# Ten query chunks laid at one stride per half, and one load of v's rows per head and half

## The reference, cut to what matters

```python
q_d, k_d, v_d = (mean over groups of 4 positions)          # 144 pooled positions
out_up = np.repeat(sm_attn(q_d, k_d, v_d), 4, axis=2)
mask = np.abs(pos[:, None] - pos[None, :]) < 4
scores = np.where(mask, scale * q @ k.T, -1e9)
out_local = softmax(scores) @ v
x = (out_up + out_local) as 1152 x 512
x = elu(x @ w_in) @ w_out                                  # 512 -> 2048 -> 512
out = sum over 4 experts e of p[:, e] * (relu(x @ w1[e]) @ w2[e])   # 512 -> 1024 -> 512
```

## Time and profile before

| | us |
|---|---|
| median of 3 runs | 653.45 (652.56 to 657.57) |
| the profiled execution | 653.07 |
| its span | 651.3 |
| PE busy | 635.3 |
| DVE / ACT / POOL busy | 348.7 / 283.2 / 321.7 |

### The profile page before, as it was taken

How to read it: one execution, slowest core, us unless ns; L and a number is a source line. 1 busy time by engine, 2 the same in 40 slices (tenths; PEclk the granted TensorE clock), 3 DMA queues, 4 the chain that set the end, 5 groups by cost and what they waited for, 6 DMA issues and landing times.

```text
span 651.3 us, 13151 instructions
## 1 busy us (share of the span) xinstructions
PE 635.3 (98%) x4775; PEld 587.2 (90%) x4775; DVE 348.7 (54%) x764; ACT 283.2 (43%) x786; POOL 321.7 (49%) x278
## 2 busy tenths in 40 slices
PE   8759999999999999999999999999999999999998
PEld 5649999999999999998998898899899899889986
DVE  5657464646557876764544454454365355365342
ACT  4667474848395686564133142152052152142210
POOL 3456444444398799899336238047056064160200
PEclk9789999999999999999999999999999999999999
DMA  8585171614122121302103003012012022010012
GB/s 168 117 218 145 49 183 30 175 33 135 66 65 105 55 99 64 130 1 82 48 2 130 1 7 123 0 53 76 0 64 64 0 64 64 0 65 2 0 49 97
DMA packets 52003, 46.10 MB, mean 71 GB/s; under 512 B 32128, under 2 KB 34432, under 8 KB 51968
## 3 DMA queue, kind: packets, MB, share of 16 engines
q1 hardware_dynamic: 50784, 45.35, 23.4%
q10 hardware_dynamic: 1184, 0.30, 0.2%
HBM read 43.27 MB, written 2.36 MB: 70 GB/s over the span
## 4 chain that ended last, share of the span: by engine, by line
PE 91%; SPq 5%; DMA 1%; ACT 1%; issue 1%; DVE 0%; DVEq 0%
PE psum L538 16%; PE psum L540 16%; PE psum L539 16%; PE psum L609 11%; PE psum L613 11%; PE psum L611 11%; PE psum L679 2%; PE psum L678 2%; PE psum L677 2%; SPq L330 2%; SPq L333 2%; DMA wa_raw<-in_moe_w_in 1%; SPq L312 1%; SPq L316 1%; PE psum L530 1%
## 5 line engine op out<-in xcount | busy, mean ns | idle before, releaser
L1635 POOL TENSOR_TENSOR wb_lo<-wb_raw,wb_hi 128x512 fp32r<-128x512 f32 x64 | 81.8, 1295 | 180.6 <-ACT wb_hi L918 180.6
L1445 DVE SCALAR_TENSOR_TENSOR o_acc<-psum,gate_now,o_acc 128x512 f32<-128x512 f32 x72 | 54.1, 751 | 126.0 <-PE psum L540 125.7
L540 PE MATMUL psum<-wb_hi,h_lo 128*128 128x512 f32 x288 | 112.3, 390 | 0.0
L539 PE MATMUL psum<-wb_lo,h_hi 128*128 128x512 f32 x288 | 112.2, 390 | 0.0
L538 PE MATMUL psum<-wb_hi,h_hi 128*128 128x512 f32 x288 | 112.0, 389 | 0.0
L1028 ACT ACTIVATE h_hi<-psum 128x320 fp32r<-128x320 f32 (+1 forms) x128 | 52.4, 411 | 87.4 <-DVE psum L1417 40.3
L1635 POOL TENSOR_TENSOR wa_lo<-wa_raw,wa_hi 128x512 fp32r<-128x512 f32 x60 | 77.5, 1318 | 16.9 <-ACT wa_hi L959 16.9
L1034 ACT COPY sums<-psum 128x256 f32<-128x256 f32 (+1 forms) x32 | 12.8, 400 | 155.2 <-PE psum L613 155.1
L613 PE MATMUL psum<-x_hi,wa_lo 128*128 128x256 f32 (+2 forms) x228 | 67.4, 296 | 0.0
L611 PE MATMUL psum<-x_lo,wa_hi 128*128 128x256 f32 (+2 forms) x228 | 67.3, 295 | 0.0
L609 PE MATMUL psum<-x_hi,wa_hi 128*128 128x256 f32 (+2 forms) x228 | 67.3, 295 | 0.0
(11 more groups left out here) (192 smaller groups left out, 1670.2 us busy)
## 6 DMA issues: line engine op xcount, KB each, us to landing
wa_raw<-in_moe_w_in SPq DMA_DIRECT2D x8, 1024.0 KB, 5.5
wb_raw<-in_moe_w_out SPq DMA_DIRECT2D x8, 1024.0 KB, 5.0
wa_raw<-in_moe_w SPq DMA_DIRECT2D x8, 1024.0 KB, 5.0
wb_raw<-in_moe_w SPq DMA_DIRECT2D x8, 1024.0 KB, 5.0
out<-o_acc SPq DMA_DIRECT2D x9, 256.0 KB, 2.0
q_in<-in_q SPq DMA_DIRECT2D x10, 144.0 KB, 5.3
v_in<-in_v SPq DMA_DIRECT2D x5, 288.0 KB
v_win<-in_v SPq DMA_DIRECT2D x20, 64.0 KB, 2.8
```

What stands on the lines that cost most here:

```text
L539: nc.tensor.matmul(bank_cols, w_hi(n), x_lo_(n), start=False, stop=False)
L540: last = nc.tensor.matmul(bank_cols, w_lo(n), x_hi_(n), start=False, stop=(n == chunks - 1))
L1445: nc.vector.scalar_tensor_tensor(o_acc[:, m, :], psum[:, DOWN2_BANKS[(MT * half + m) % 2], :], gate_now[:, m:m + 1], o_acc[:, m, :], ALU.m ...
L1635: nc.gpsimd.tensor_tensor(lo[:, c, :], raw[:, c, :], hi[:, c, :].bitcast(F32), ALU.subtract).then_inc(lo_ready, 1)
```

## The change

The five windows of each half now all begin at the same distance of 58. `WIN_SECOND`, 280, is where the second half's first window begins, and the last one ends at 576 exactly. The first chunk of the first half takes 61 tokens, since nothing lies before position 0, the last of the second half 61 as well, and their neighbours at the middle 53 each (tokens 235 to 287, and 288 to 340). The other six keep 58. The places that a chunk's output takes in PSUM follow from its tokens (`at`). Since all five windows of a half fit one access pattern, `load_v` issues four window DMAs of 64 x 5 rows in place of eight, and the wait in `mix` goes by 64 in place of 128.

```diff
-TOK_AT = [HALF * (s % 2) + QSTEP * (s // 2) for s in range(NQT)]
-TOK_N = [min(QSTEP, HALF - QSTEP * (s // 2)) for s in range(NQT)]
-Q_AT = [min(t, SEQ - QT) for t in TOK_AT]
-WIN_AT = [min(max(t - FACTOR + 1, 0), SEQ - WIN) for t in TOK_AT]
+WIN_SECOND = SEQ - WIN - QSTEP * (CHUNKS - 1)
+WIN_AT = [WIN_SECOND * (s % 2) + QSTEP * (s // 2) for s in range(NQT)]
+Q_AT = [0 if s == 0 else min(WIN_AT[s] + FACTOR - 1, SEQ - QT) for s in range(NQT)]
+TOK_AT = [HALF * s if s < 2 else WIN_AT[s] + FACTOR - 1 for s in range(NQT)]
+TOK_N = [(TOK_AT + [HALF, SEQ])[s + 2] - TOK_AT[s] for s in range(NQT)]
...
-                for e, (i0, odd) in enumerate(((1, 0), (0, CHUNKS - 1))):
-                    part = slice(WIN * e, WIN * (e + 1))
+                for e in range(2):
                     for h in range(2):
-                        at = rows.offset + h * SEQ * HD
-
-                        sp.dma_start(win[part, i0:i0 + CHUNKS - 1, h, :],
-                                     bass.AP(rows.tensor, at + WIN_AT[2 * i0 + e] * HD,
-                                             [[HD, WIN], [QSTEP * HD, CHUNKS - 1], [1, HD]])).then_inc(win_loaded[held(u)], 16)
-                        sp.dma_start(win[part, odd, h, :],
-                                     bass.AP(rows.tensor, at + WIN_AT[2 * odd + e] * HD, [[HD, WIN], [1, HD]])
-                                     ).then_inc(win_loaded[held(u)], 16)
+                        sp.dma_start(win[WIN * e:WIN * (e + 1), :, h, :],
+                                     bass.AP(rows.tensor, rows.offset + (h * SEQ + WIN_SECOND * e) * HD,
+                                             [[HD, WIN], [QSTEP * HD, CHUNKS], [1, HD]])).then_inc(win_loaded[held(u)], 16)
...
-                pe.wait_ge(win_loaded[held(u)], 128 * loads(u))
+                pe.wait_ge(win_loaded[held(u)], 64 * loads(u))
...
-                        rows = slice(WIN * e, WIN * (e + 1))
+                        rows, at = slice(WIN * e, WIN * (e + 1)), TOK_AT[c] - HALF * e
...
-                        last = nc.tensor.matmul(psum[HD * h:HD * (h + 1), banks[e], QSTEP * i:QSTEP * i + TOK_N[c]],
+                        last = nc.tensor.matmul(psum[HD * h:HD * (h + 1), banks[e], at:at + TOK_N[c]],
```

## The result

| | before | changed |
|---|---|---|
| median, us | 653.45 (652.56 to 657.57) | 643.73 (643.49 to 643.83) |
| profiled execution, us | 653.07 | 643.81 |
| its span | 651.3 | 642.0 |
| PE busy | 635.3 | 632.8 |

Both medians are now of five executions. The ratio is 0.9846, with a 95% interval of 0.9817 to 0.9876: 9.7 us by the medians, 9.3 us by the two profiled executions. The forecast was 642.3, in a range of 640.0 to 646.8.

A forecast was written before the change was run, and what follows sets the result against it. SP's issuing was taken to bound the first 45 us, PE the rest. Gains of 4.7 + 5.2 + 1.3 = 11.2 us took the profiled 653.07 to 641.9, a median of 642.3, range 640.0 to 646.8.

The forecast's parts named there:

- What binds: Claim that SP's issuing, not a computing engine, bounds the first 45 us, and PE bounds the kernel after that.
- The price of an issue: SP's queue: each new window DMA of 64 x 5 rows takes 0.67 us to issue, bounds 0.57 and 1.34.
- Term A: Up to ACT's `x_hi`: pair 3's q in time, PE's 3.0 us wait and lower clock gone, ACT 4.7 us earlier.
- Term B: At ACT's first weight cast: `wa_raw` lands before ACT wants it, so its whole 5.2 us wait goes; at worst 3.
- Term C: Behind the first weight cast: PE's clock stays up for the products and `mix(3)`; 1.3 us, between 0 and 1.6.
- The sum: Whole kernel: 4.7 + 5.2 + 1.3 = 11.2 us gained, for a median of 642.3 us.
- the signs that the prediction named: Profile after: issues 0.67 us apart, `wa_raw` issued at 26 to 28, `first_wa(0)` near 35, no q wait, full clock.
- Rival 1: First stage: transfers bind, not issues; `wa_raw` lands at 37 to 40, gain 6 to 9 us; chance 0.13.
- Rival 2: SP's queue: a 64 x 5 issue costs what two did, 1.34 us, so time stays 653; chance 0.07.
- Rival 3: `load_v` ahead of `wa_raw`: five-window transfers stall SP, slower, 664 us at 2.0 us an issue; chance 0.03.

The follow-up runs named there:

- experiment 1: Changed kernel's new chunks, but each half's windows loaded in two DMAs again, eight a pair: 653.60 us against 653.72 for the kernel before.
- experiment 2: Changed kernel with window loads merged only for pairs 0 and 1 and the mixed pairs, those of pairs 2 and 3 in eight DMAs: 650.44 us, before 653.72.
- experiment 3: Changed kernel with window loads merged only for pairs 2 and 3, those of pairs 0, 1 and the mixed pairs in eight DMAs: 647.78 us, before 653.72.
- experiment 4: The changed kernel itself once more, with no edit: 643.75 us against 653.72 for the kernel before.
- experiment 6: Changed kernel with the first weights issued ahead of pair 3's v: 643.74 us against 652.90 for the kernel before.
- experiment 9: Changed kernel with ten filling products at the start in place of eight: 644.16 us against 652.92 for the kernel before.
- experiment 7: Changed kernel with window loads of pairs 1 to 3 cut to one window of five, same number of issues: 643.03 us, before 652.90.
- experiment 11: Kernel before with the first weights issued ahead of pair 3's v, pair 4's q and k last: 648.61 us against 652.92 unedited.
- experiment 5: Kernel before with 32 products of zeros behind pair 4's k transposes, keeping PE busy while it waits for the first weights: 651.36 us against 652.90.

## Why the prediction was right

**What binds.** Shown. SP's issuing bound the first stage: in experiment 1 the gain is gone with nothing changed but the issues, and from 60 to 500 us PE is as full as it was. The sixteen issues saved behind the first weights lie beside a full PE, and the equal rests of experiments 2 and 3 agree; no run took them back alone.

**The price of an issue, 0.67 us.** Right for three of the four groups ahead of the weights; the fourth took 3.51 us with the gap, 0.88 each. Together, long ones included, the window issues ahead of the weights went from 23.5 to 11.5 us. That the other issues would get longer was missed: those of q, k and `v_in` grew by 3.3 us, so the weights were issued 8.7 us earlier (29.55 against 38.22) and not 10.7.

**Term A, 4.7 us.** The mechanism was right: PE no longer stood for pair 3's q and went on at full clock. It was mis-sized as a total: ACT came to the weights at 36.82 in place of 39.84, 3.0 us earlier. The step that failed is the one that took everything up to 21.58 us as unchanged: in one profile the clock rose late, in two (the slowest executions of experiments 4 and 6) a k of pair 2 was late. Where neither happened, ACT was ready at 35.50 in experiment 9 and cast at 35.16 in experiment 7, which is term A at 4.3 and 4.7.

**Term B, 5.2 us.** The wait is gone, but the reason given for it held only in part. The weights were to land at 33.3 to 34.3, a microsecond ahead of ACT. They landed at 36.75, because they were issued 2.0 us later than forecast and took 7.2 in place of 6.8 us, and nothing was left of the margin. Term B came out whole because ACT was late as well, which is luck: in experiment 9 ACT was in time and waited 1.36 us. Experiment 11 has the mechanism in the kernel before, at 4.3 us.

**Term C, 1.3 us.** Right: 1.1 by the rests of the two profiles (606.3 and 605.2), 1.5 by experiment 5. The six products and `mix(3)` took 2.33 in place of 3.98 us, 1.65 less, and began 2.66 in place of 2.06 us behind the cast. The prediction had PE come to the last `x_lo` just as it ended, 8.3 us behind the cast, a figure that its rows do not give; in the profile that `x_lo` ended 8.4 us behind it, and PE did not wait for it. Term C is larger where the clock comes back late: 607.5 to 607.9 in experiments 1 to 3, 2.3 to 2.7 us over the changed kernel.

**The sum.** 3.0 + 5.2 + 1.1 = 9.3, the difference of the two spans. 11.2 was forecast; the 1.7 us of term A and 0.2 of C are the miss. They can't be laid to the late start alone, since with the weights landing at 36.75 an earlier ACT would have waited and term B would have been the short one. Of the signs that the prediction named, two did not come: `wa_raw` was issued at 29.55 and not at 26 to 28, and ACT's cast began at 36.82 and not near 35. The others came.

**Rival 1** was given 0.13 as an alternative. It turned out to be beside the forecast and not in its place: the share went to 1.15 and 0.99 where 0.79 was worked out, and the loads of pair 2's and 3's q landed 4.8 us behind their issue (median) in place of 3.0. From 10 to 20 us the bytes moved grew by the factor expected, from 127 to 184 GB/s, but the share doubled. That packets waiting for one another each count for longer would explain it and is not shown. A share of 0.57 did not mean that 0.43 more was free. The Trainium skill's sentence in "DMA: Bandwidth & Descriptors", section "Issuing engines are not separate DMA queues", that the time to initiate a DMA is usually small relative to the DMA itself, agrees with the trace for a single load: a window of 64 x 4 rows took 0.62 us to issue and landed 2.9 us after its issue (medians of the kernel before, up to 40 us). What does not follow from it is that a merge is worth nothing. The issues stand one behind another while the transfers overlap, and in experiment 1 against experiment 4 the same rows in twice the window issues cost 9.9 us. In the changed kernel the transfers may bind too; but experiment 7, with a fifth of the window rows in three pairs, was not shown to be faster, so that they bind it alone is not shown either.

**Rivals 2 and 3** are excluded by the issue times.

## What to carry to other kernels

When one engine only issues transfers, read its queue as an engine of its own: if it has no gap from the start to the load that everyone waits for, each issue is on the path, and halving their number pays up to the next limit, here two at once, the landing of the weights and ACT's own work, 0.1 us apart. When two limits meet like this, taking away one alone may show nothing. What the merge is worth depends on which issues stand ahead of which landing, so count them ahead of each wait and not in the whole program. And where a wait of PE goes, count the time at the lower clock behind it as part of the wait.

## What was not expected of the hardware

- Two issues of q (96 x 6 rows of 256 B each) took 1.13 us in the kernel before at 10.61 us and 1.69 to 1.98 us in the changed kernel, with the DMA share at 1.0 and above; three of four groups of window issues stayed at 0.67 us each with the gap. A long one also came at a share near 0.6: 2.21 us for pair 3's q in the kernel before.
- The granted clock reads 1.00 from 5 to 10 us in the changed kernel's first profile, while 12 products that take 0.95 us at full clock took 1.51. In that profile the column could not be relied on at the start; the durations could.
- An idle time of PE of 1.24 us left the clock up, one of 2.04 us behind other short ones (experiment 9) was followed by the lower clock, 0.71 in the mean from 38.2 to 50 us. The waits of 1.99 and 1.63 us for pair 2's k in experiments 4 and 6 were followed by a clock of 0.50 too, from 19 us to about 22 us in both.
